# A first MLP whose first product goes by Strassen's blocks for the 512-token chunks

## The reference

```python
h = x @ w_in                     # 2304 x 512 by 512 x 2048
g = h - np.tanh(h)
x = g @ w_out                    # 2048 x 512
h = x @ w2_in                    # 512 x 1024
e = np.exp(h - np.max(h, axis=-1, keepdims=True))
solu = h * (e / (np.sum(e, axis=-1, keepdims=True) + 1e-09))
mu = np.mean(solu, axis=-1, keepdims=True)
var = np.mean((solu - mu) ** 2, axis=-1, keepdims=True)
out = ((solu - mu) / np.sqrt(var + 1e-06) * g_ln) @ w2_out
```

## Time and profile before

| | before |
|---|---|
| median of 3 runs | 809.47 us |
| profiled execution: own time | 809.84 us |
| profiled execution: span, first to last instruction | 808.0 us |
| PE busy | 796.7 us (99%) |
| DVE busy | 465.2 us (58%) |
| ACT busy | 395.9 us (49%) |
| POOL busy | 274.5 us (34%) |

### The profile page before, as it was taken

One profiled execution on the slowest core, in us unless ns is written; L12 is line 12 of the kernel. 1 busy time (PEld: TensorE's weight loads), 2 busy tenths in 40 slices (PEclk: granted clock), 3 DMA queues, 4 the chain that ended last, 5 costly groups with the idle time before them and its releaser, 6 DMA issues. The chain is left out here.

```text
span 808.0 us, 14647 instructions
## 1 busy us (share of the span) xinstructions
PE 796.7 (99%) x4532; PEld 670.1 (83%) x4532; DVE 465.2 (58%) x1100; ACT 395.9 (49%) x935; POOL 274.5 (34%) x323
## 2 busy tenths in 40 slices
PE   8999999999999999999999999999999999999998
PEld 7788888888888899988888888888887788888886
DVE  5888999897954343422233222443568666666661
ACT  5999999998544242322223222443344344433342
POOL 4778877877100000000000000016553754444400
PEclk9999999999999999999999999999999999999999
DMA  7655556553523200000000000002000000000001
GB/s 178 165 148 151 144 154 162 151 141 119 160 93 101 79 1 1 2 0 1 1 0 0 0 0 0 1 1 104 1 1 0 27 27 27 26 26 13 25 14 53
DMA packets 77723, 46.40 MB, mean 57 GB/s; under 512 B 59824, under 2 KB 68144, under 8 KB 77680
## 3 DMA queue, kind: packets, MB, share of 16 engines
q1 hardware_dynamic: 75232, 45.19, 19.6%
q10 hardware_dynamic: 2448, 0.66, 0.4%
HBM read 40.97 MB, written 4.87 MB: 57 GB/s over the span
## 5 line engine op out<-in xcount | busy, mean ns | idle before, releaser
L1465 PE MATMUL psum<-x_hi,w1i 128*128 128x512 f32 (+1 forms) x640 | 182.0, 369 | 0.0
L1478 PE MATMUL psum<-gate_hi,w1o 128*128 128x512 f32 (+1 forms) x640 | 146.0, 370 | 0.0
L1465 PEld LDWEIGHTS psum<-x_hi,w1i 128*128 128x128 f32 x640 | 115.4, 188 | 20.6 <-DVE w1i L1119 0.4
L1478 PEld LDWEIGHTS psum<-gate_hi,w1o 128*128 128x128 f32 x640 | 112.4, 188 | 21.1
L1162 DVE TENSOR_TENSOR gate_lo<-gate,gate_hi 128x512 fp32r<-128x512 f32 (+1 forms) x80 | 53.6, 670 | 125.0 <-ACT gate_hi L869 125.0
L1465 PE MATMUL psum<-x_lo,w1i 128*128 128x512 f32 (+1 forms) x320 | 117.7, 368 | 0.0
L711 POOL TENSOR_TENSOR w2t<-stage 128x512 f32<-128x512 f32 x2 | 4.3, 2164 | 327.9 <-DVE w2x L1136 327.9
L869 ACT ACTIVATE gate_hi<-gate 128x512 fp32r<-128x512 f32 (+1 forms) x80 | 47.2, 590 | 134.7 <-PE psum L1478 126.5
L1150 DVE TENSOR_TENSOR gate<-psum,gate 128x512 f32<-128x512 f32 (+1 forms) x80 | 51.0, 638 | 95.8 <-ACT gate L856 94.2
L856 ACT ACTIVATE gate<-psum 128x512 f32<-128x512 f32 (+1 forms) x80 | 44.4, 555 | 111.7 <-PE psum L1465 90.8
L894 ACT ACTIVATE probs<-probs,neg_max 128x128 f32<-128x128 f32 (+2 forms) x144 | 83.6, 586 | 9.5 <-DVE neg_max L1195 9.3
(11 more groups left out here) (159 smaller groups left out, 1410.4 us busy)
## 6 DMA issues: line engine op xcount, KB each, us to landing
cum_bc<-cum_dram SPq DMA_DIRECT2D x16, 576.0 KB, 4.6
rden_T<-rden_dram SPq DMA_DIRECT2D x32, 144.0 KB, 3.0
out_x<-out_sb SPq DMA_DIRECT2D x18, 256.0 KB, 2.0
stage<-in_q SPq DMA_DIRECT2D x32, 128.0 KB, 2.4
v_raw<-in_v SPq DMA_DIRECT2D x32, 128.0 KB, 3.7
stage<-in_moe_w_in SPq DMA_DIRECT2D x16, 256.0 KB, 3.0
stage<-in_moe_w_out SPq DMA_DIRECT2D x16, 256.0 KB, 3.3
stage<-in_k SPq DMA_DIRECT2D x28, 128.0 KB, 2.3
```

Source lines behind the costliest of these rows:

```text
L1465: mm = pe.matmul(h_ps[j % 4][:, 0:wide(c)], wp[j][:, kt, :], xp[:, kt, 0:wide(c)], start=(n == 0), stop=(n == 3 * KT - 1))
L1478: mm = pe.matmul(y_ps[m][:, 0:wide(c)], wp[j][:, m * P:(m + 1) * P], gp[j % 2][:, 0:wide(c)], start=(j == 0 and wp is w1o_hi and gp is gat ...
```

## The change

The 2048 inner rows are done in two halves of eight tiles. The order of the chunks is `CHUNKS`; its first entry is done as before with eight steps, and the nine others are called runs 0 to 8, of four groups each (`GROUPS` = 36, group g is pair g % 4 of run g // 4; a group makes two inner tiles).

- A group of a 512-token run (28 of them) makes its two tiles by 7 products of 6 matmuls with 256 columns, into three banks. DVE adds five block sums from PSUM into h_blocks, ACT copies two. The 256-token chunk (runs 0 and 5) keeps 24 plain matmuls of 256 columns for a group.
- PE runs products(g), downs(g - 1), products(g + 1). downs is 24 matmuls as before.
- x's sums S1 to S4 and the lo parts of seven blocks are made on DVE and the hi parts on ACT, during the run before; into other places in every second run, so that they can be early.
- w_in's sums are made on POOL, and split on ACT and DVE; the second half's weights are loaded and split in groups 13 to 17.
- y of the first half goes to DRAM (`y_dram`) for four chunks, comes back, and is added on DVE and POOL in the second half.
- The second MLP's w2 sums move from POOL to DVE (groups 32, 33 and 35), the splits of w2_in's blocks go to groups 34 and 35, and the split of w2_out goes to the start of the second MLP.
- split_y of the second MLP uses another order with 10 steps for 12; the places in SBUF are laid out anew.

```diff
+    FT1 = FT // 2
+    CHUNKS = [0, 1, 2, 3, 4, 4, 1, 0, 2, 3]
...
-    W2_AT = {"B21": 0, "T4": 2, "T2": 4, "T1": 6, "T3": 8, "B22": 12, "B11": 14}
...
-    W2_STEP = {"B22": 2, "B11": 3, "B21": 5, "T4": 9, "T2": 10, "T1": 11, "T3": 13}
...
-    W2O_STEP = {12: (0, 1), 14: (2, 3, 4, 5), 15: (6, 7)}
...
+    PAIRS1 = FT1 // 2
+    GROUPS = PAIRS1 * (len(CHUNKS) - 1)
+    LAST_GROUP = GROUPS - 1
...
     PRODUCTS = [("A11", "B11", 0), ("S2", "T2", 1), ("S1", "T1", 2), ("A12", "B21", 0), ("S3", "T3", 1), ("S4", "B22", 2), ("A22", "T4", 1)]
...
+            def pair_sums(n):
...
+                pool.tensor_tensor(t1, b12, b11, ALU.subtract).then_inc(w1b_summed, 1)
+                pool.tensor_tensor(t3, b22, b12, ALU.subtract).then_inc(w1b_summed, 1)
...
+                pool.tensor_tensor(t2, b22, t1, ALU.subtract).then_inc(w1b_summed, 1)
...
+                pool.tensor_tensor(t4, b21, t2, ALU.subtract).then_inc(w1b_summed, 1)
...
+            pool.wait_ge(pair_product, products_before(GROUPS))
+            pool.wait_ge(w2i_lo_done, W2_NTH["T3"] + 1)
             split_y(1, 1)
```

ACT's loop over the groups, in part:

```diff
+            for g in range(GROUPS):
...
+                if short(run):
+                    if pair == 1:
+                        copy_y(run)
+                    for t in range(2):
+                        tanh(g, t)
+                        gate_high(g, t)
+                    for name in (("A11",), ("S1", "S2", "S4"), ("A12", "S3"), ("A22",))[pair]:
+                        x_hi_part(ahead, name)
+                    if run == 0 and pair >= 2:
+                        pair_sums_hi(pair - 2)
+                else:
+                    copy_first(g)
+                    if pair == 1:
+                        copy_y(run)
+                    copy_c11(g)
+                    if run == 1 and pair < 2:
+                        pair_sums_hi(pair + 2)
...
+                    later_weights(g)
+                    if g == LAST_GROUP - 1:
+                        for name in ("T1", "T2", "T4"):
+                            w2i_hi_part(name)
+                    tanh(g, 0)
...
+                    gate_high(g, 0)
+                    if g == LAST_GROUP:
+                        w2i_hi_part("T3")
+                    tanh(g, 1)
+                    if g == LAST_GROUP:
+                        w2i_hi_part("B22")
+                    gate_high(g, 1)
+                    if g == LAST_GROUP - 1:
+                        w2i_hi_part("B11")
+                        w2i_hi_part("B21")
```

ACT at the start of the second MLP:

```diff
+            copy_p1(0, 2)
+            for f in range(4):
+                w2o_hi_part(f)
+            exp2(0, 0, 2)
+            w2o_hi_part(4)
+            w2o_hi_part(5)
+            exp2(0, 1, 2)
+            copy_y(len(CHUNKS) - 1)
             normalise(0, 0)
+            w2o_hi_part(6)
+            w2o_hi_part(7)
             copy_p1(1, 1)
```

DVE's loop over the groups, in part:

```diff
+            for g in range(GROUPS):
...
+                if short(run):
+                    if pair == 1:
+                        copy_half(run, 2)
+                        copy_half(run, 3)
+                    for t in range(2):
+                        gate_of(g, t)
+                        gate_low(u + t, 2 * n)
+                    for name in (("S1", "S2"), ("S4", "S3"), (), ())[pair]:
+                        x_block_sum(ahead, name)
+                    for name in ((), ("S1",), ("S2", "A11", "S4", "A12"), ("S3", "A22"))[pair]:
+                        x_block_low(ahead, name)
+                    if run == 0 and pair >= 2:
+                        pair_sums_lo(pair - 2)
+                    continue
...
+                keep_first(g, 2, 1, 2)
+                keep_first(g, 3, 2, 3)
+                if pair == 1:
+                    copy_half(run, 2)
+                    copy_half(run, 3)
...
+                block_sum1(g, 5, 1, 3)
+                if blocks and pair == 3:
+                    x_block_sum(ahead, "S3")
+                block_sum1(g, 6, 2, 2)
+                block_sum1(g, 7, 1, 1)
+                if g == LAST_GROUP:
+                    w2_sums("T3")
+                gate_of(g, 0)
...
+                if weights:
+                    pair_lo(later, 0)
+                if g == LAST_GROUP - 1:
+                    w2i_lo_part("T1")
+                if g == LAST_GROUP:
+                    w2i_lo_part("B11")
+                gate_low(u, 2 * n)
...
+                if g == LAST_GROUP - 1:
+                    w2i_lo_part("T2")
+                if g == LAST_GROUP:
+                    w2i_lo_part("B21")
+                gate_of(g, 1)
...
+                if weights:
+                    pair_sums_lo(later)
+                if g == LAST_GROUP - 1:
+                    w2i_lo_part("T4")
+                if g == LAST_GROUP:
+                    w2i_lo_part("T3")
+                gate_low(u + 1, 2 * n)
+                if run == 1 and pair < 2:
+                    pair_sums_lo(pair + 2)
+                if ahead is not None and short(ahead) and pair == 2:
+                    short_x_lo(ahead)
+                if PAIRS1 <= later - 1 < 2 * PAIRS1:
+                    for j in range(2):
+                        w1o_lo_later(2 * (later - 1 - PAIRS1) + j)
+                if g == GROUPS - PAIRS1:
+                    w2_sums("T1")
+                if g == GROUPS - PAIRS1 + 1:
+                    w2_sums("T2")
+                    w2_sums("T4")
+                if g == LAST_GROUP:
+                    w2i_lo_part("B22")
```

PE:

```diff
+            def products(g):
...
+                    elif nth == 0:
+                        pe.wait_ge(c11_copied, blocks_before(g))
+                    elif nth < 3:
+                        pe.wait_ge(block_summed, 5 * blocks_before(g))
+                    elif nth == 3:
+                        pe.wait_ge(first_copied, blocks_before(g) + 1)
+                    elif nth < 6:
+                        pe.wait_ge(block_summed, 5 * blocks_before(g) + nth - 3)
+                    else:
+                        pe.wait_ge(block_summed, 5 * blocks_before(g) + 3)
...
+            products(0)
+            first_down(FT1 - 1)
+            for g in range(1, GROUPS):
+                products(g)
+                downs(g - 1)
```

More of the change, by code:

```diff
@@ new lines, in short, with blocks_before, products_before, split_run @@
+        def short(run):
+            return wide(CHUNKS[run + 1]) < CH
+        def blocks_before(g):
+            return sum(not short(n // PAIRS1) for n in range(g))
+        def products_before(g):
+            return 7 * blocks_before(g) + 2 * (g - blocks_before(g))
+        SPLIT_RUNS = [run for run in range(len(CHUNKS) - 1) if CHUNKS[run + 1] != CHUNKS[run]]
+        BLOCK_RUNS = [run for run in SPLIT_RUNS if not short(run)]
+        def split_run(run):
+            return run if run in SPLIT_RUNS else run - 1
@@ new lines, in place, with x_free @@
+        def place(run, name):
+            return name in XB_TWO and SPLIT_RUNS.index(split_run(run)) % 2 == 0
+        def x_free(eng, run, name):
+            for before in range(run - 1, -1, -1):
+                if short(before) and place(run, name):
+                    eng.wait_ge(pair_product, products_before(PAIRS1 * (before + 1)))
+                    return
+                if not short(before) and place(before, name) == place(run, name):
+                    eng.wait_ge(pair_product, products_before(PAIRS1 * (before + 1) - 1) + XB_AT[name] + 1)
+                    return
+            eng.wait_ge(up_done, FT1)
@@ new lines, in x_block, with x_of, x_part @@
+        def x_block(run, name):
+            at, n = tokens(CHUNKS[run + 1]).start, wide(CHUNKS[run + 1]) // 2
+            first, half = int(name[1]) - 1, int(name[2]) - 1
+            return xT[:, HK * half:HK * half + HK, at + first * n:at + first * n + n]
+        def x_of(parts, run, name):
+            if not place(run, name):
+                return parts[0][:, XB_AT[name], :, :, :]
+            n = XB_TWO.index(name)
+            return parts[1 + n // 2][:, n % 2, :, :, :]
+        def x_part(run, name, part):
+            return x_of((x_blocks, x_other_a, x_other_b), run, name)[:, part, :, :]
@@ L721, in split_y, with add_y @@
+            def add_y(e):
+                k, c = e - NCH, CHUNKS[e]
+                pool.wait_ge(y_act, 2 * (e + 1))
+                wait(pool, y_back, 16 * k)
+                own = xT[:, 0:HK, tokens(c)]
+                pool.tensor_tensor(own, own, y_half[:, 0:HK, 0:wide(c)], ALU.add).then_inc(y_added, 1)
             def split_y(i, par):
@@ new lines, in gate_high, with copy_y @@
+            def gate_high(g, t):
+                run, pair, n = group(g)
+                u = FT1 + 2 * g + t
+                act.wait_ge(gate_done, u + 1)
+                act.wait_ge(down_done, u - 1)
+                act.activation(gate_hi[t][:, 0:2 * n], gate[:, 0:2 * n], ACT.Copy).then_inc(gate_hi_done, 1)
+            def copy_y(e):
+                act.wait_ge(down_done, FT1 * (e + 1))
+                if 0 < e < NCH:
+                    act.wait_ge(y_stored, 16 * e)
```

(22 more changed lines are left out.)

798 lines of the change are left out of this document (544 added, 254 removed).

## The result

The changed kernel takes **842.23 us** (median of 4 runs, 840.67 to 842.75), the kernel before 809.54 on the same chip. The ratio is 1.0399, with a 95% interval from 1.0386 to 1.0412: slower by 32.7 us. 825 was forecast with a range to 836, so the side was right, but the sum was 17 us short, and the time lies above the range.

What follows compares the result with a forecast made beforehand. PE, busy 99% of the span, was taken as the bound. A gain of 13.7 us against added costs A to H gave +15.6, from 809.84 to 825 us; range 805 to 836, likeliest case 813 to 833.

Steps and rivals of the forecast that it cites:

- The gain: Products of 28 block groups: 42 matmuls of 256 columns take 4.99 us instead of 5.48, saving 13.7 us in all.
- Rival 4: 256-column matmuls with hand-overs every six cost as much as before: no gain, 839 us; chance 6%.
- C: Groups 4 to 6, after the 256-token chunk's first pass: queued low parts and splits delay DVE's first sum; 3.9 us.
- H: Last group and second MLP's start: DVE's queue of sums, splits and low parts makes PE wait; 8.5 us.
- Rival 1: Hand-overs have more slack than the 0.75 us read, so C to H shrink: 806 or 802 us; chance 17%.
- E: After the 256-token chunk's second pass, and short_x_lo in group 18: queued DVE work delays the sum; 1.1 us.
- B: y's copies: 0.1 us more each in block groups, 0.75 us each in the two short runs; 2.2 us.
- G: End of group 34: four strided high parts on ACT delay the copy of product 1; 4.0 us.
- A: Seventh product of all 28 block groups waits for DVE's sum, 0.07 us each; 2.0 us (0 to 5.6).
- Term F: w2 sums on DVE: strided sums queued in groups 32 and 33 delay the first sum; 4.8 us.
- rival 3: POOL blocks DVE in more places (groups 32, 33, add_y, all of H): 10 us more, 835 us; chance 12%.
- D: Second half's weights: low parts on DVE around gate_lo delay the first sum, three times 0.78, once 0.45; 2.8 us.

Runs made afterwards that it cites:

- e1: Changed kernel with the seventh product of the 28 block groups in a bank of its own, waiting for no sum (computation incomplete): 837.6 us.
- r2: e2 with the high parts B11 and B21 on ACT moved from the end of group 34 into group 35: 828.35 us.
- c1: Changed kernel with PE made to wait for POOL memsets before product 3 in groups 7, 9 and 11 (0.26, 0.66, 1.14 us): 845.77 us.
- e3: Changed kernel with 24 unused matmuls put into each of PE's three waits in groups 33, 34 and 35: 838.04 us.
- h2: Changed kernel with r2's and r3's edits, the first MLP's weight-sum low parts moved on DVE, and w2_out's low parts left out: 819.93 us.
- r3: Changed kernel with the first matmul of the following downs issued between products 6 and 7 in 21 groups: 840.58 us.
- e2: Changed kernel with the second MLP's weight sums T1, T2, T4 and T3 moved from DVE back to POOL: 834.99 us.
- c2: As c1, but each memset waits for the one before, making waits of 4.04, 5.62 and 7.17 us: 863.5 us.

## Why the prediction was right in its side and short in its size

**The gain** stood: e1's groups have 0.118 to 0.120 us a matmul. Rival 4 (no gain by 256 columns) falls.

**One number, 0.75 us of DVE's slack,** was to carry C to H. Rival 1 (more slack) falls: the waits came in groups 4, 5, 6, 15 to 19, 33, 34 and 35, with the releasers named, and E, B and G were met within 0.2 us. r2 takes 5.07 us out of group 35, G and the clock behind it.

**The step that failed is the sum's lack of a term for what a wait does afterwards.** I took PE's rate as 0.119 whatever stood before. The waits themselves were nearly right. B to H cost 41.8 us, the sum of the table. Their waits are 29.9, which is 28.8 more than the kernel before has in the second MLP (1.1), and 27.3 was forecast. So of the 17.3 us that the sum lacks, 1.5 are longer waits, 2.8 are A, and 13.0 are what the waits brought with them. There are two parts to it. Each wait costs 0.25 to 0.3 us beyond itself (c1), and behind some the granted clock falls to 0.50. e3 gives the clock's price: 3.0 us in groups 33 and 34. In group 4 it is some 1.3 us: the same two waits there (1.65 and 0.45) made a group of 9.00 us in the changed kernel and of 7.66 in r2, where the clock stayed at 1.00. In the second MLP it is 1.1 on balance (from up2(0) to the end 840.9 - 615.7 = 225.2 us, and 827.0 - 602.9 = 224.1 in r2, whose clock stayed at 1.00). Together that is about 5 of the 17 us.

Counted where they stand, the slow stretches of the second MLP cost more than this 1.1. The transposes and the first 12 matmuls behind the wait for act, in the changed kernel and then in r2:

```profile
663.10 1.75 PE L2313 MATMUL psum<-ident,act 128*128 128x128 f32 x8 [2.17 <-ACT act L1366]
664.49 4.09 PE L2330 MATMUL psum<-w2o,lnT 128*128 128x512 f32 x12
```

```profile
649.73 1.09 PE L2311 MATMUL psum<-ident,act 128*128 128x128 f32 x8 [2.15 <-ACT act L1393]
650.58 3.01 PE L2328 MATMUL psum<-w2o,lnT 128*128 128x512 f32 x12
```

They take 5.3 us (to 668.42) against 3.7 (to 653.43), and up2(1) loses another 1.3 to 1.7 the same way. But r2, which is early there, then waits 0.80 us twice where the changed kernel does not: a slow stretch swallows waits that would have come next.

**Term F was mis-sized** (4.8, measured 12.2), and is the largest miss. The price of a strided sum, which had no row, was right: 2.11 for two against my 2.1. So was the wait in group 34 (3.12; 3.45 forecast). Wrong was that the reach of POOL's work, which the prediction left open, stood in the sum at nothing: T1 took 4.31 for 2.1 beside POOL's add_y, and split_y(0) of 12 us slowed DVE ahead of group 32:

```profile
557.23 1.22 DVE L1585 TENSOR_TENSOR gate<-h_blocks,gate 128x512 f32<-128x512 f32 x1
557.86 1.20 POOL L960 TENSOR_TENSOR y_raw<-xT,y_raw 128x256 f32<-128x256 f32 x1
559.53 1.52 DVE L1563 TENSOR_TENSOR gate_lo<-gate,gate_hi 128x512 fp32r<-128x512 f32 x1
```

Both DVE operations take 0.69 elsewhere, and PE waits 1.05 us in group 32. That is rival 3 in two places: 2.2 us in group 33 and 1.6 in group 32 (6.79 against 5.16). No run took POOL's work away there, so these two shares are read from the rows. The clock makes another 3.0.

**Term A** (2.0, measured 4.8) was mis-sized on PE's side. Product 7 starts 4.37 us into the group, and 4.35 was forecast, so the hand-over itself was read rightly. But it was due at 4.24 and not 4.28, and its own six matmuls then took 0.78 and not 0.71. That was inside the bounds named (0 to 5.6), near their upper end.

**Terms C and D** (6.7, measured 11.0): besides group 4's clock, each wait lengthens its group by 0.25 to 0.3 us more than itself; c1 shows that alone (0.26 to 0.51, 0.66 to 0.97, 1.14 to 1.38). In D the first sum came 3.6 us into the group, and 3.06 was forecast.

**Term H** (8.5, measured 11.6): of the six waits forecast four are there (1.58, 1.65, 2.54, 1.23), two are not (copy_p1(1) and down2(0)), and one is that I had not seen, 2.17 for act ahead of the second turn; it was 0.82 before. All waits come to 9.2 us against 1.1 before, so 8.0 more where 8.5 was forecast; that the two agree is in part luck, since the single ones do not. The slow stretches make about 3 more. h2 shows that DVE's low parts hold 3.5 us of H. For the other 8 I have shown no single cause.

**The sum again.** 15.6 + 2.8 + 4.3 + 7.4 + 3.1 is 33.2, less 0.3 in B and G: 32.9.

**What stays open.** Which wait makes the clock fall. In the traces here none up to 1.49 us did by itself, and those of 3.56 and more always. In between the same wait did in one run and not in another: 1.64 with 0.46 behind it in group 4 did in the changed kernel and not in e1, r2 and r3; 2.54 did in the changed kernel (0.64 behind it) and 2.52 did not in r2 (1.00); 3.43 in group 35 did in e1, e2 and c2 and not in the changed kernel. What decides there was not tried.
